# Evicting a transposed probability tile in one piece instead of two halves

## The reference

```python
# 2 batches x 8 heads, 768 rows, 64 columns, 16 clusters
mask = q_assign[:, :, :, None] == k_assign[:, :, None, :]
scores = scale * np.matmul(q, k.transpose(0, 1, 3, 2))
scores = np.where(mask, scores, -1000000000.0)
scores = scores - np.max(scores, axis=-1, keepdims=True)
attn = np.exp(scores)
attn = attn / (np.sum(attn, axis=-1, keepdims=True) + 1e-09)
return np.matmul(attn, v)
```

## Time and profile before

| what | value |
|---|---|
| median of 3 runs | 712.58 us |
| the profiled execution's own time | 712.5 us |
| its span | 710.7 us |
| TensorE matmuls busy | 679.5 us, 96% |
| VectorE busy | 418.0 us, 59% |
| ScalarE busy | 331.6 us, 47% |
| GpSimd busy | 226.4 us, 32% |
| first transposes of tile 0, last tile 95 | 25.3 us, 281.4 us |

### The profile page before, as it was taken

One profiled execution on the slowest core, in us unless ns is written; L12 is line 12 of the kernel. 1 busy time (PEld: TensorE's weight loads), 2 busy tenths in 40 slices (PEclk: granted clock), 3 DMA queues, 4 the chain that ended last, 5 costly groups with the idle time before them and its releaser, 6 DMA issues.

```text
span 710.7 us, 11568 instructions
## 1 busy us (share of the span) xinstructions
PE 679.5 (96%) x4154; PEld 642.3 (90%) x4154; DVE 418.0 (59%) x697; ACT 331.6 (47%) x641; POOL 226.4 (32%) x164
## 2 busy tenths in 40 slices
PE   3899999999999998999999999999997999999998
PEld 3788898989898887889999999999996999999998
DVE  7498979888898988345202303412389834783133
ACT  3687878787978788524401201302345504421010
POOL 5549352534535374302500000100175502461000
PEclk9999999999999999999999999999999899999999
DMA  6364735435353451101300000100411100000022
GB/s 211 70 155 125 182 78 139 112 88 133 66 133 66 99 145 44 45 1 46 104 0 1 1 1 0 44 0 1 125 53 47 59 0 1 1 1 1 0 84 95
DMA packets 16016, 45.44 MB, mean 64 GB/s; under 512 B 2544, under 2 KB 4592, under 8 KB 15984
## 3 DMA queue, kind: packets, MB, share of 16 engines
q1 hardware_dynamic: 15984, 45.00, 23.4%
HBM read 24.15 MB, written 3.15 MB: 38 GB/s over the span
## 4 chain that ended last, share of the span: by engine, by line
PE 83%; DVE 11%; issue 3%; ACT 2%; DMA 0%; DVEq 0%; ACTq 0%
PE ps L457 17%; PE ps L458 17%; PE ps L459 17%; PE ps L494 7%; PE ps L502 5%; PE ps L486 4%; PE ps L503 4%; PE ps L487 4%; PE ps L467 3%; PE ps L478 2%; DVE pt_lo L1056 2%; PE ps L509 1%; DVE turn L1165 1%; DVE neg_max L1028 1%; DVE z_s L1170 1%
## 5 line engine op out<-in xcount | busy, mean ns | idle before, releaser
L1028 DVE TENSOR_REDUCE neg_max<-ps 128x1 f32<-128x768 f32 x96 | 91.5, 953 | 25.7 <-PE ps L487 22.8
L1056 DVE TENSOR_TENSOR pt_lo<-ps,pt_hi 128x384 fp32r<-128x384 f32 x192 | 97.4, 548 | 11.5 <-ACT pt_hi L758 11.1
L758 ACT ACTIVATE pt_hi<-ps 128x384 fp32r<-128x384 f32 x192 | 84.5, 489 | 38.0 <-PE ps L494 36.6
L783 ACT ACTIVATE prob<-ps,neg_max 128x768 f32<-128x768 f32 x96 | 86.8, 905 | 13.9 <-DVE neg_max L1028 12.6
L867 ACT ACTIVATE g_s<-ps 128x384 fp32r<-128x384 f32 x48 | 23.6, 492 | 139.4 <-PE ps L459 139.4
L459 PE MATMUL ps<-u_s,ch_s 128*128 128x384 f32 (+1 forms) x256 | 85.5, 334 | 0.0
L457 PE MATMUL ps<-u_s,ch_s 128*128 128x384 f32 (+1 forms) x256 | 85.5, 334 | 0.0
L458 PE MATMUL ps<-u_s,ch_s 128*128 128x384 f32 (+1 forms) x256 | 85.5, 334 | 0.0
L494 PE MATMUL ps<-ident,prob 128*128 128x128 f32 x576 | 83.1, 278 | 1.4 <-DVE pt_lo L1056 1.3
L494 PEld LDWEIGHTS ps<-ident,prob 128*128 128x128 f32 x576 | 66.8, 143 | 11.2 <-DVE pt_lo L1056 3.2
L502 PE MATMUL ps<-pt_lo,v_s 128*128 128x384 f32 x192 | 70.1, 365 | 4.8 <-DVE o_sum L1035 4.8
(11 more groups left out here) (142 smaller groups left out, 1516.1 us busy)
## 6 DMA issues: line engine op xcount, KB each, us to landing
stage<-ch_dram SPq DMA_DIRECT2D x9, 768.0 KB, 4.4
qa<-pair_s SPq DMA_DIRECT2D x30, 192.0 KB, 3.0
ka<-pair_s SPq DMA_DIRECT2D x30, 192.0 KB, 3.8
raw<-q_dram SPq DMA_DIRECT2D x8, 384.0 KB, 4.2
raw<-k_dram SPq DMA_DIRECT2D x8, 384.0 KB, 4.5
raw_v<-v_dram SPq DMA_DIRECT2D x8, 384.0 KB, 4.2
out_dram<-act_u SPq DMA_DIRECT2D x16, 192.0 KB, 1.9
qb<-pair_s SPq DMA_DIRECT2D x15, 192.0 KB, 3.4
```

The source lines that it names most:

```text
L758: return act.activation(o, i, ACT.Copy)
L783: act.activation(prob[:, slot, :].rearrange("p (c k) -> p c k", c=2), ps[:, 2 * slot:2 * slot + 2, 0:HS], ACT.Exp, bias=neg_max[:, s:s + 1 ...
L1028: dve.tensor_reduce(neg_max[:, s:s + 1], ps[:, 2 * slot2:2 * slot2 + 2, 0:HS], AX.XY, ALU.max, negate=True).then_inc(s_max, 1)
L1056: dve.tensor_tensor(pt_lo[at], ps[:, 4 + u, 0:HS].rearrange("p (k q) -> p k q", k=HT), pt_hi[at], ALU.subtract).then_inc(s_pt_lo, 1)
```

## The change

The copy on ScalarE and the subtraction on VectorE take the 768 columns of both banks in one instruction each. `s_pt`, `s_pt_hi` and `s_pt_lo` step once per tile, and all waits on them are renumbered. The amount of data is the same.

```diff
-            def transposes(g, slot, u):
+            def transposes(slot):
-                for i in range(HT):
-                    mm = pe.transpose(ps[:, 4 + u, i * P:(i + 1) * P],
-                                      prob[:, slot, (HT * u + i) * P:(HT * u + i + 1) * P], ident[:])
+                for u in range(2):
+                    for i in range(HT):
+                        mm = pe.transpose(ps[:, 4 + u, i * P:(i + 1) * P],
+                                          prob[:, slot, (HT * u + i) * P:(HT * u + i + 1) * P], ident[:])
                 mm.then_inc(s_pt, 1)
...
                     pe.wait_ge(s_exp, g + 1)
-                    for u in range(2):
-                        if not (first and s == 0):
-                            pe.wait_ge(s_pt_lo, 2 * g + u - 1)
-                        transposes(g, s % 2, u)
+                    if not (first and s == 0):
+                        pe.wait_ge(s_pt_lo, g)
+                    transposes(s % 2)
...
-                    for u in range(2):
-                        act.wait_ge(s_pt, 2 * g + u + 1)
-                        copy(pt_hi[:, half, HT * u:HT * u + HT, (t % HT) * P:(t % HT + 1) * P],
-                             ps[:, 4 + u, 0:HS].rearrange("p (k q) -> p k q", k=HT)).then_inc(s_pt_hi, 1)
+                    act.wait_ge(s_pt, g + 1)
+                    at = pt_hi[:, half, :, (t % HT) * P:(t % HT + 1) * P].rearrange("p (u k) q -> p u k q", u=2)
+                    copy(at, ps[:, 4:6, 0:HS].rearrange("p u (k q) -> p u k q", k=HT)).then_inc(s_pt_hi, 1)
...
-                    for u in range(2):
-                        dve.wait_ge(s_pt_hi, 2 * g + u + 1)
-                        at = (slice(None), half, slice(HT * u, HT * u + HT), slice((t % HT) * P, (t % HT + 1) * P))
-                        dve.tensor_tensor(pt_lo[at], ps[:, 4 + u, 0:HS].rearrange("p (k q) -> p k q", k=HT),
-                                          pt_hi[at], ALU.subtract).then_inc(s_pt_lo, 1)
-                        if not last and u == 1 and 3 <= s <= 7:
-                            argmax(p + 1, s - 3)
+                    dve.wait_ge(s_pt_hi, g + 1)
+                    lo, hi = (w[:, half, :, (t % HT) * P:(t % HT + 1) * P].rearrange("p (u k) q -> p u k q", u=2)
+                              for w in (pt_lo, pt_hi))
+                    dve.tensor_tensor(lo, ps[:, 4:6, 0:HS].rearrange("p u (k q) -> p u k q", k=HT), hi,
+                                      ALU.subtract).then_inc(s_pt_lo, 1)
+                    if not last and 3 <= s <= 7:
+                        argmax(p + 1, s - 3)
```

More of the change, by code:

```diff
@@ L566, in pair @@
                     if prev and t < 2:
-                        pe.wait_ge(s_pt_lo, 6 * n - 1 + t)
+                        pe.wait_ge(s_pt_lo, 3 * n)
                         if t == 0:
@@ L571, in pair @@
                     if t in (3, 4):
-                        pe.wait_ge(s_pt_lo, 6 * n + 5 + t - 3)
+                        pe.wait_ge(s_pt_lo, 3 * n + 3)
                         if t == 3:
@@ L596, in _ @@
             pair(NP - 1, last=True)
-            pe.wait_ge(s_pt_lo, 12 * 2 * NP)
+            pe.wait_ge(s_pt_lo, NG)
             pe.wait_ge(s_x_bank, 4 * NP - 1)
@@ L636, in _ @@
                     if n < 2:
-                        pe.wait_ge(s_pt_lo, 2 * NG)
+                        pe.wait_ge(s_pt_lo, NG)
                     elif n == 2:
@@ L796, in pair @@
                         if not (first and s == 0):
-                            act.wait_ge(s_pt, 2 * g)
+                            act.wait_ge(s_pt, g)
                         exp(g + 1, (s + 1) % 2, (s + 1) % 12)
```

## The result

The changed kernel takes 752.22 us (751.39 to 753.27, 4 runs) against 712.56 us for the kernel before measured beside it. The ratio is 1.0558, with a 95% interval of 1.054 to 1.0577: the change costs 39.7 us. The forecast was 743 with a range of 731 to 754.

The account below looks back on a forecast made before the run. TensorE was taken as the bound, VectorE and ScalarE close behind. Seven pairs +24.6, the last pair +5.6 and last value matmuls +0.5 gave +30.7 us; 710.7 span plus this plus 1.8 gave 743 us, range 731 to 754.

Parts of the forecast that it names:

- heavy and light steps: One step per tile of a pair; heavy ones, with value matmuls, took about 2.40 us, the light one without them 1.85.
- step 5: Step of a pair without value matmuls: from 1.85 us up to the loop's 2.78, +0.93 us.
- The loop's length: Per tile, six transposes 0.88, copy 0.80, subtraction 0.95 and hand-overs 0.04, 0.06, 0.05: 2.78 us, minimum for a step.
- the hand-overs: Delays between engines in the loop: to ScalarE 0.04 us, to VectorE 0.06, back to TensorE 0.05.
- 3, 4, 7, 8, 10, 11: Six steps of a pair, together 14.38 us, were to take 2.78 each, 16.68: +2.30 us.
- 0: Step following a `half_out`, set by VectorE's own queue: 2.89 us against 2.44, +0.45 us.
- 6: Step following a `half_out`, set by VectorE's own queue: 2.97 us against 3.14, -0.17 us.
- the last pair: Pair without `sims` or `argmax` and with fewer scores: eleven steps from 25.74 to 31.30 us, +5.6.
- VectorE paces the stage: Rival: VectorE is the true bound, so 0.06 us saved per tile comes through 96 times, 707 us; chance 0.03.
- TensorE's other work covers most of it: Rival: loop comes out at 2.40 us, so only steps without value matmuls lose, 719 us; chance 0.05.
- ScalarE comes late too: Rival: a late exponential delays the copy 0.3 us in the four `o_t` copy steps per pair, 753 us; chance 0.10.
- The clock falls: Rival: short new waits bring TensorE's clock from 2.4 to 1.2 GHz in the pairs, 920 us; chance 0.01.

Follow-up runs that it names:

- less TensorE work: The changed kernel without the 192 value matmuls of `pt_lo`: 751.56 us.
- more VectorE work: The changed kernel with one extra 384-column VectorE instruction behind the subtraction in four steps of each pair: 754.76 us.
- four partial changes: The kernel before with whole copy alone, whole subtraction alone, one TensorE wait per tile, or copies after all six transposes: 733.92, 732.67, 723.53, 724.04 us.
- one wait for halves: The kernel before, halves everywhere, except that TensorE waits once for both halves of the tile before: 723.53 us.
- Without the add: VectorE's add of 1e-9 to the denominators left out, reciprocal reading them directly: changed kernel 745.49 us, kernel before 710.01 us.

## Why the prediction was right, and where it was short

*The mechanism.* The prediction's heart was that the loop transposes, copy, subtraction, transposes runs once per tile and sets every step shorter than itself. The changed trace shows it: heavy and light steps alike take 2.83. The kernels with less TensorE work (751.56) and with more VectorE work (36.65 per pair) show that neither engine's work paces these steps; ScalarE's was not varied, but it stood idle 0.76 us in front of the copy in the turn shown above. Three of the four partial changes land on their own loops: 2.50, 2.57, 2.17 against 2.50, 2.53, 2.17 worked out beforehand. The fourth, one wait for halves, does not: its loop of 2.15 was to show in step 5, which took 2.31. There the copy began 0.70 behind the first load, where 0.59 was priced, since TensorE had not been waiting. The whole copy costs 1.9 us per pair and the whole subtraction 1.65; their sum, 3.55, is near the 3.98 of both together.

*The loop's length.* 2.78 was forecast, 2.83 measured. The copy (0.81 for 0.80) and the subtraction (0.96 for 0.95) were right; the hand-overs were 0.03, 0.03 and 0.12 instead of 0.04, 0.06 and 0.05. The last of the three was the one mis-sized: I read it behind the second of two half subtractions. In the kernel with one wait, where TensorE also waits for the whole tile but the subtraction is in halves, it is 0.05 (176.45 to 176.50); in the kernel with the whole subtraction alone it is 0.12 (163.26 to 163.38). So it goes with the instruction of 768 columns and not with the coarse wait; why was not tested.

*The steps.* The forecast against what was measured, in us, from a pair in the middle of either kernel (those that begin at 123.94 and 176.61), where no held add lengthens a step:

| steps of a pair | forecast | measured |
|---|---|---|
| 3, 4, 7, 8, 10, 11 | +2.30 | +2.96 (14.38 to 17.34) |
| 5 | +0.93 | +0.98 |
| 0 | +0.45 | +0.39 |
| 6 | -0.17 | -0.18 |
| 1 | 0 | -0.12 |
| 9 | 0 | -0.04 |
| a pair | +3.51 | +4.0 |

The first row is the loop's 0.05 six times, and steps 3, 7 and 10 at 2.98, 2.90 and 2.96. In steps 3 and 10 TensorE had not been waiting, and a tile whose transposes follow directly on other matmuls ends them 0.96 to 1.00 behind its first load instead of 0.88. The prediction gave 0.88 for a TensorE that has been waiting and priced all six steps at it. In step 3 the copy also starts 0.10 behind the transposes instead of 0.03; it has a second wait in front of it there (`s_pv`), as in steps 6 and 9, where it is 0.09 and 0.10, but also in step 0, where it is 0.03. In step 7 the subtraction starts 0.11 behind the copy; it has a second wait in front of it there (`s_oh_t`), and in the last pair, where that is absent, the step takes 2.83. Whether the second wait is the cause in either place was not tested.

*The sum.* Without the add in both kernels the change costs 745.49 - 710.01 = 35.5 us, where 30.7 was forecast. The two traces place the difference. Six pairs (1 to 6) cost 4.0 each instead of 3.5, which is the mechanism with the mis-sized terms above, 3.2 us. Pair 0 costs 5.5, 2.0 over the forecast: the six transposes of its first tile took 1.54 us in both kernels, and the whole copy waits for all of them, and without the add those of the second tile took 1.51 as well. The prediction had priced this pair like the others. The last pair costs 6.2 instead of 5.6. The remaining 4.2 us of the 39.7 are what the add costs more in the changed kernel (752.22 - 745.49 = 6.7) than before (712.54 - 710.01 = 2.5). The step of the prediction that was short here is the statement that row maxima and `half_out` behind a subtraction keep their length, 2.02 and 1.94 us. They did in the pair that I read; I had not looked at all 32 of the small adds, of which five were already held before, for 0.31 to 1.51 us. In the changed kernel one add is held in each middle pair too, 0.80 us in step 2, where it costs nothing. No end of the stated range allowed for a held add. That 752.22 still lies inside it is luck: the range was made from the spread of the copy and the subtraction, and these came out as forecast.

*The rivals.* "VectorE paces the stage" is excluded by the test with more VectorE work, and "TensorE's other work covers most of it" by the loop's length and by the test with less TensorE work. "ScalarE comes late too" did not come about: the copy starts 0.03 or 0.04 behind the transposes in the four steps with an `o_t` copy. Its cover had left out the copies of 768 columns into `qb` and `kb` in steps 0, 1, 8 and 9; behind them ScalarE stood idle only 0.17 and 0.23 us before the next tile's copy, in steps 1 and 9. "The clock falls" I had at 920 us and a chance of 0.01. It did not fall in the pairs with short waits; it fell for some 3.4 us behind the one wait of 3.21 us, which cost 1.5 us in one step (4.45 against 2.93). The 920 us stood for a clock at half all along; what the cited section tells of is a swing between the two levels, and that would cost less. Neither came.

*The rules of the Trainium skill.* Of the two in Perfetto Trace Analysis, "Optimizing Scalar/DVE Operations", the one on breaking up operations was the one to follow here. The grouping saved 5.5 us of VectorE's busy time (97.4 to 91.9), not the 12 estimated from the page's figure, and none of it reached the end.

## What to carry to other kernels

An instruction on the way between two engines costs its full length to whoever waits for it, so an eviction in two halves that overlaps with the work at both its ends can be worth more than the overhead of the second instruction: here 6 us of busy time saved on each of two engines cost 35 us. Before merging, add up one turn of the loop through all engines and compare it with what the bound engine has to do in one turn, the shortest one first. And look for small instructions of one engine that are held until a long one of another ends: moving anything can make them meet.

## What the runs showed of the hardware that was not expected

- A VectorE instruction of three columns that reads only SBUF was held until a running GpSimd `tensor_tensor` ended, for up to 3.44 us (in the kernel with more VectorE work), as `tensor_scalar` with one input and as `tensor_tensor` with two. A reciprocal of one input, and all instructions that read PSUM for one of their inputs, were not held. The Trainium skill (SBUF — State Buffer, "Who interferes with whom") says that VectorE and GpSimd share a pair of SBUF ports: a VectorE instruction in a two-port mode, which `tensor_scalar` can enter, needs the pair, and one with two SBUF inputs needs its read side, against GpSimd instructions that read SBUF. The traces agree with it (3.35 and 3.36 us against 0.16).
- A wait of TensorE of 3.21 us was followed by some 3.4 us at 1.2 GHz, with matmuls of 384 columns at 0.52 us; waits of 0.2 to 1.0 us in most steps, and one of 1.74, left it at 1.00 from 72 to 320 us. In the partial changes it fell in the last pair too, behind waits of 2.41 to 3.13 us.
